# Sparse attention and two feed-forward layers on one core: paired first units, and mask, sums and scaling in other steps

## The reference

```
scores = q @ k.T / 8
mask   = scores >= the 32nd largest score of the row
attn   = softmax of the kept scores over each row
out    = attn @ v
```

```
x1 = leaky(x @ w_in1) @ w_out1     leaky(h) = max(0.01 h, h)
x2 = bump(x1 @ w_in2) @ w_out2     bump(h) = 0 below -1, h above 1, (h + 1)^2 / 4 between
```

## Time and profile before

| what | value |
|---|---|
| median of 3 runs (lowest, highest) | 1286.73 us (1286.48, 1287.85) |
| the profiled execution's own time | 1285.5 us |
| its span | 1283.6 us |
| mean granted TensorE clock | 0.949 |
| TensorE busy, share of the span | 1128.7 us, 88% |
| VectorE busy | 910.8 us, 71% |
| ScalarE busy | 700.2 us, 55% |
| GpSimd busy | 640.9 us, 50% |
| DMA | 287.12 MB, mean 224 GB/s |

### The profile page before, as it was taken

One profiled execution on the slowest core, in us unless ns is written; L12 is line 12 of the kernel. 1 busy time (PEld: TensorE's weight loads), 2 busy tenths in 40 slices (PEclk: granted clock), 3 DMA queues, 4 the chain that ended last, 5 costly groups with the idle time before them and its releaser, 6 DMA issues.

```text
span 1283.6 us, 21057 instructions
## 1 busy us (share of the span) xinstructions
PE 1128.7 (88%) x7360; PEld 1010.6 (79%) x7360; DVE 910.8 (71%) x2056; ACT 700.2 (55%) x1577; POOL 640.9 (50%) x614
## 2 busy tenths in 40 slices
PE   3334699888999989989999998999899999999998
PEld 1222488777988878878888877888788899999997
DVE  7976897989989889899996997987989201100111
ACT  4454477665657666576665754765766423322232
POOL 5454577873347454466434753543745324432343
PEclk9755699899999999999999998999999999999999
DMA  6675598777666668667866665554445667687763
GB/s 237 231 254 181 192 343 296 251 252 249 215 218 202 213 216 300 235 228 240 271 225 221 215 207 175 185 193 153 148 179 171 210 231 259 233 270 253 245 224 127
DMA packets 86504, 287.12 MB, mean 224 GB/s; under 512 B 9600, under 2 KB 13184, under 8 KB 86400
## 3 DMA queue, kind: packets, MB, share of 16 engines
q1 hardware_dynamic: 78912, 270.04, 61.5%
q10 hardware_dynamic: 7488, 15.73, 3.6%
HBM read 247.46 MB, written 38.27 MB: 223 GB/s over the span
## 4 chain that ended last, share of the span: by engine, by line
PE 62%; DVE 9%; ACT 8%; POOL 6%; issue 4%; ACTq 0%; POOLq 0%
PE ps_f L730 47%; PE ps_av L695 6%; POOL gate L575 4%; DVE top L934 3%; DVE work L937 2%; PE ps_s L651 2%; PE ps_t L672 2%; PE ps_t L651 2%; DVE part_r L961 2%; ACT probs L803 2%; ACT gate L865 1%; PE ps_t L678 1%; ACT part_o L855 1%; ACT part_r L854 1%; ACT probs L795 1%
## 5 line engine op out<-in xcount | busy, mean ns | idle before, releaser
L730 PE MATMUL ps_f<-gate,w_ring 128*128 128x384 f32 (+2 forms) x2688 | 435.2, 319 | 21.9 <-POOL gate L575 21.9
L730 PEld LDWEIGHTS ps_f<-gate,w_ring 128*128 128x128 f32 x2688 | 412.2, 192 | 40.9 <-POOL gate L575 24.6
L730 PE MATMUL ps_f<-xy,w_ring 128*128 128x384 f32 (+2 forms) x2688 | 431.0, 316 | 8.6 <-POOL xy L585 5.5
L730 PEld LDWEIGHTS ps_f<-xy,w_ring 128*128 128x128 f32 x2688 | 407.2, 190 | 26.6 <-issue 13.4
L934 DVE MAX8 top<-work 128x8 f32<-128x576 f32 x432 | 310.0, 744 | 0.1
L560 POOL TENSOR_TENSOR drop<-scores,drop 128x576 f32<-128x576 f32 x144 | 207.6, 1442 | 125.7 <-DVE drop L943 125.7
L937 DVE MATCH_REPLACE8 work<-top,work 128x576 f32<-128x576 f32 x288 | 213.6, 742 | 0.0
L575 POOL TENSOR_TENSOR gate<-part_r,gate 128x384 fp32r<-128x384 f32 (+2 forms) x112 | 101.0, 904 | 169.4 <-ACT gate L859 169.3
L965 DVE TENSOR_TENSOR y_acc<-ps_f,y_acc 128x384 f32<-128x384 f32 (+2 forms) x56 | 27.8, 497 | 208.2 <-PE ps_f L730 208.2
L961 DVE SCALAR_TENSOR_TENSOR part_r<-part_r 128x384 f32<-128x384 f32 (+2 forms) x112 | 72.3, 645 | 115.6 <-ACT part_o L855 115.3
L795 ACT ACTIVATE probs<-drop,neg_max 128x576 f32<-128x576 f32 x144 | 112.4, 781 | 62.6 <-issue 45.6
(11 more groups left out here) (79 smaller groups left out, 1290.6 us busy)
## 6 DMA issues: line engine op xcount, KB each, us to landing
w_ring<-w_split SPq DMA_DIRECT2D x412, 512.0 KB, 4.1
w_split<-w_ring SPq DMA_DIRECT2D x36, 512.0 KB, 5.5
raw<-wd SPq DMA_DIRECT2D x64, 256.0 KB, 3.9
w_split<-xy SPq DMA_DIRECT2D x28, 512.0 KB, 2.9
kq<-kqd ACTq DMA_DIRECT2D x12, 576.0 KB, 5.4
v_sb<-vd ACTq DMA_DIRECT2D x12, 320.0 KB, 3.9
kq<-kqd SPq DMA_DIRECT2D x4, 576.0 KB, 6.9
out_t<-y_acc ACTq DMA_DIRECT2D x12, 192.0 KB, 4.5
```

Source lines behind the costliest of these rows:

```text
L730: mm = pe.matmul(out, ww, xx, start=a == 0, stop=a == count - 1)
```

## The change

Six things are changed.

1. In `make_plan`, where the next unit waits for the unit just before it, it and the next one are marked `paired` and always put in one step. `feed` then runs such a pair in turn: all source blocks but the last of the first unit, all but the last of the second, then the last of the first, then the last of the second. The order of the three matmuls of a source block and their number stay.
2. GpSimd: in steps before 22 the mask goes first; the direct pieces and the low halves come one step later than before, behind mask and low_x. From step 22 on the mask keeps its place between the first and the second group.
3. SyncE: the raw loads and the stores of prepared pieces are issued one step later in its list. ScalarE's high halves stay.
4. VectorE: the items of the first four pairs close one turn earlier (before, only those of the fourth), and `close_sum` stands ahead of `find_drop`.
5. ScalarE: `normalise` goes ahead of the exponential in steps before 22; from then on it is done one step early, between the first and second group.
6. Scores of mixed items beyond tile 20 are made one step earlier.

```diff
 def score_step(it):
-    return max(0, it.first - 2) if it.first <= 20 else it.first
+    if it.first <= 20:
+        return max(0, it.first - 2)
+    return it.first - it.mixed
...
-            credit -= queue[0].ns
-            now.append(queue.pop(0))
-        cut = [a for a in range(1, len(now)) if waits_for(now[a], now[a - 1])]
-        first = cut[0] if cut else (len(now) + 2) // 3
-        second = first + (len(now) - first + 1) // 2
+            both = last is not None and waits_for(queue[0], last)
+            for u in queue[:1 + both]:
+                credit -= u.ns
+                u.paired = both
+                now.append(u)
+            last = now[-1]
+            del queue[:1 + both]
+        opens = [a for a in range(1, len(now)) if now[a].paired and waits_for(now[a], now[a - 1])]
+        first = opens[0] if opens else (len(now) + 2) // 3
+        second = first + max((len(now) - first + 1) // 2, 2 * bool(opens))
+        if second < len(now) and now[second].paired and now[second].i:
+            second += 1
...
-        if it.last + INV_LAG - (it.gp == CHUNKS[0].last_gp) == t:
+        if it.last + INV_LAG - starts_early(it.gp) == t:
...
@@ SyncE @@
-                for a in direct_pieces(s):
+                for a in direct_pieces(s - 1):
                     load_raw(a + RAW_SLOTS)
-                for i in prep_pieces(s):
+                for i in prep_pieces(s - 1):
                     store_split(i)
                     load_raw(JOB_OF[PREP[i]] + RAW_SLOTS)
...
@@ GpSimd @@
-                for u in first:
-                    event(u)
-                for a in direct_pieces(s):
-                    low_direct(a)
-                for i in prep_pieces(s)[:1]:
-                    low_piece(i)
-                if 0 <= s - MASK_LAG < TILES:
+                if s < READY[0] and s >= MASK_LAG:
                     mask(s - MASK_LAG)
                 if s - 1 in VALUES_AT and s < READY[0]:
                     low_x(VALUES_AT[s - 1])
-                for i in prep_pieces(s)[1:]:
+                for a in direct_pieces(s - 1):
+                    low_direct(a)
+                for i in prep_pieces(s - 1):
                     low_piece(i)
+                for u in first:
+                    event(u)
+                if READY[0] <= s < TILES + MASK_LAG:
+                    mask(s - MASK_LAG)
...
@@ TensorE, feed @@
+                if u.paired and u.i:
+                    return
+                open_bank(u)
+                if not u.paired:
+                    products(u, range(u.sources))
+                    return
+                other = UNITS[u.n + 1]
+                products(u, range(u.sources - 1))
+                open_bank(other)
+                products(other, range(other.sources - 1))
+                products(u, [u.sources - 1])
+                products(other, [other.sources - 1])
...
@@ ScalarE @@
+                if done and s < READY[0]:
+                    normalise(done)
                 if s < READY[0] and 0 <= s - EXP_LAG:
                     exponential(s - EXP_LAG)
...
-                if done:
-                    normalise(done)
...
+                if s + 1 in OUT_AT and s >= READY[0]:
+                    normalise(OUT_AT[s + 1])
                 for u in second:
                     event(u)
...
@@ VectorE @@
+                if shut:
+                    close_sum(shut)
+                    count += 1
                 if old:
                     dve.wait_ge(dve_step, last_top)
                     find_drop(t - 1)
                 if shut:
-                    close_sum(shut)
-                    count += 1
                     dve.wait_ge(dve_step, count)
                     invert_sum(shut)
```

More of the change, by code:

```diff
@@ L143 @@
     needs: int = -1
+    paired: bool = False
     @property
@@ L155, in ns, with sources @@
         return 3 * (CK if self.hidden else BLOCK_F) * (self.width / 2.4 + 12)
+    @property
+    def sources(self):
+        return CK if self.hidden else BLOCK_F
     @property
@@ L214, in make_plan @@
     queue, at, led = [], 0, 0
-    plan, credit = [], 0.0
+    plan, credit, last = [], 0.0, None
     for s in range(ATTENTION_STEPS + 1):
@@ L696, in values, with open_bank @@
                 mm.then_inc(av_done, 1)
-            def feed(u):
+            def open_bank(u):
                 if u.n >= BANKS:
@@ L706, in feed @@
                     pe.wait_ge(scores_copied, 2 * SCORED_EARLY)
-                count = 3 * (CK if u.hidden else BLOCK_F)
-                a = 0
                 if u.hidden and u.i == 0 and not u.layer and not u.block:
                     pe.wait_ge(x_low_done, u.chunk.last_gp + 1)
-                for g in u.pieces:
-                    if g in DIRECT:
-                        pe.wait_ge(low_split, JOB_OF[g] + 1)
-                    else:
[L715 to L731, removed]
@@ L732, in feed, with products @@
-                mm.then_inc(unit_done, 1)
+            def products(u, some):
+                for b in some:
+                    piece = 0 if u.hidden else b // F_PER_PIECE
+                    g = u.pieces[piece]
+                    if b == piece * F_PER_PIECE:
+                        if g in DIRECT:
+                            pe.wait_ge(low_split, JOB_OF[g] + 1)
+                        else:
+                            pe.wait_ge(w_loaded[g % W_SLOTS], 16 * (LOADS_BEFORE[g] + 1))
+                    m = slice((b - piece * F_PER_PIECE) * P, (b - piece * F_PER_PIECE + 1) * P)
+                    w = w_ring[:, g % W_SLOTS, :, :]
+                    if u.hidden:
+                        if u.layer and not u.block and u.i == 0:
+                            pe.wait_ge(y_low_done, Y_OF[u.chunk.n, b].y + 1)
+                        high, low, out = x_of(u.chunk, 0, b), x_of(u.chunk, 1, b), as_x(u.chunk, bank(u))
+                    else:
+                        source = GATE_OF[u.segment, b]
+                        if u.i == 0:
+                            pe.wait_ge(gate_low_done[u.layer], source.in_layer + 1)
+                        high, low, out = gate[:, 0, source.slot, 0:u.width], gate[:, 1, source.slot, 0:u.width], bank(u)
+                    end = b == u.sources - 1
+                    pe.matmul(out, w[:, 0, m], high, start=b == 0, stop=False)
+                    pe.matmul(out, w[:, 0, m], low, start=False, stop=False)
+                    mm = pe.matmul(out, w[:, 1, m], high, start=False, stop=end)
+                if end:
+                    mm.then_inc(unit_done, 1)
@@ new lines, in feed @@
+            def feed(u):
+                if u.paired and u.i:
[10 more added lines that the diff above has]
+                products(other, [other.sources - 1])
```

## The result

The changed kernel takes 1250.33 us (median of 4 runs, 1249.73 to 1252.43) beside 1287.29 us for the kernel before (4 runs, 1286.48 to 1288.33): a ratio of 0.9715, 95% interval 0.9699 to 0.9732, 37 us less. Forecast were 1249 us, 1234 to 1268. The profiled execution took 1249.73 us, with a span of 1247.7 and a mean clock of 0.953.

What follows compares the result with a forecast made beforehand. The opening was taken as latency-bound with no full engine, the rest as nearly full. Terms −30 −3.7 +4 −5 −3 = −37.7 took 1285.5 to 1247.8 us, 1249 us as a median; range 1234 to 1268.

Steps and rivals of the forecast that it cites:

- The opening: Stretch before the first main unit: start 33 us earlier, less 3 us for late raw loads, so −30 us.
- the rival of the transfers: Opening held by its transfers or raw slots, 327 of 338 GB/s: gain 17 us instead of 30, 1262 us; chance 0.15.
- the step that gave the gain to the mask's place: Opening: a weight piece ahead of the mask holds the exponential; closing item 7 earlier adds nothing at the end.
- The sum for ScalarE's chain: Opening: ScalarE's work for four tiles sums to 22.9 us, 5.7 us a turn, against 5.45 that VectorE needs.
- Lock between find_drop and low halves: Opening: VectorE and GpSimd lock each other out; costed at 0, up to 20 us; as rival 1262 us, chance 0.07.
- The 1.71 us: Opening: one find_drop beside four low halves took 1.71 us against 0.51 alone, taken as evidence of the lock.
- Pairs: Middle and end: 17 pairs hide waits ahead of last source blocks, −3.7 us, and cost +4 us on VectorE.
- catching up comes out of its own waits: VectorE, held at a pair's first addition, makes it up from existing waits; seven pairs 0 to +38 us, taken +4.
- Scaling half a step earlier: Middle: TensorE's 9.4 us of waits for scaled probabilities shrink where ScalarE was late, −5 us.
- The slower rival: Scaling between ScalarE's first and second group waits for VectorE's closing at 72 places; at 1 us each 1321 us; chance 0.04.
- Mixed scores: Middle: TensorE's 3.2 us of waits ahead of mixed scores, behind the copy of the last transposes, go: −3 us.

Runs made afterwards that it cites:

- run 3: Kernel before with both opening changes only (mask first, pieces one step later, early closings, scaling first): 1256.76 us, ratio 0.9758.
- run 2: Kernel before with early items closed one turn earlier and scaling ahead of the exponential before step 22, mask not moved: 1257.83 us, ratio 0.9773.
- run 5: Changed kernel without pairs, planner and feeding of units as before: 1244.28 us, ratio 0.9666.
- run 11: Changed kernel with pairs in the last step alone and scores of mixed items back in their old step: 1240.49 us, ratio 0.9644.
- run 12: On top of run 11, every last-step output stretch opens with a pair and the second layer puts off three source blocks: 1233.4 us, ratio 0.9588.
- run 9: Changed kernel with pairs in the last step alone and scaling from step 22 on back at the head of its own step: 1255.19 us, ratio 0.9761.
- runs 10: Changed kernel with scores of mixed items back in their old step, all else as changed: 1247.88 us, ratio 0.9695.
- run 1: Kernel before with only the mask ahead of the low halves and pieces one step later on GpSimd and SyncE before step 22: 1260.92 us, ratio 0.9797.

## Why the prediction was right

The total was right, and it came from one large term that was right in size and three small ones whose errors cancelled.

*The opening: right in size, half right in cause.* The forecast had the first unit 33 us earlier and took 3 off for raw loads: 30. It was 29.1 us earlier, at 122.57, and run 3 gives 30.8 us of time for these parts alone. The closing of item 7 came at 110.59, where 107.5 was forecast. The raw loads cost about what was foreseen: ScalarE waited for them in six pieces, 7.0 us in all and up to 2.8 at once, where 0 to 1.5 a piece was forecast. The DMA share rose to 0.78, so the rival of the transfers fell. Its ceiling had been read too low: 338 GB/s is not the busiest stretch of before, which moved 378 GB/s from 184 to 192 us. But the step that gave the gain to the mask's place, and nothing at the end to closings and scaling, failed: run 2 has 29.7 us without moving the mask. The sum for ScalarE's chain was made with both parts in, and so could not tell them apart.

*Lock between find_drop and low halves: nearly absent in the new order.* In the row of all 17 find_drops from 20 to 120 us (min, median and max in ns) the median is 508. The longest, 1274, starts at 54.80, beside low halves that a late `low_x` had pushed back to 54.48.

```profile
L979 DVE TENSOR_SCALAR drop<-scores,top x17: 504/508/1274, 22.5 to 116.1; 128x576 f32<-128x576 f32 x17
```

The term, taken at 0, holds; by the Trainium skill's rule (SBUF — State Buffer, "Who interferes with whom") that is what an order without overlap gives. The 1.71 us of the kernel before were misread in the prediction: GpSimd's four low halves end at 22.04, and what the find_drop of 22.00 ran beside is the mask of the tile before it:

```profile
22.00 1.39 POOL L560 TENSOR_TENSOR drop<-scores,drop 128x576 f32<-128x576 f32 x1
```

The find_drop of 15.79 us, 1.42 us long, is beside a low half.

*Pairs: wrong.* Forecast 3.7 won less 4 lost; measured 6.0 lost (run 5). The term that failed is the cost on VectorE, "catching up comes out of its own waits": its waits for units grew instead, by 8 to 10 us, and 7.6 to 11.1 us were lost in the attention steps. The gain there failed too: the waits for low parts of first-layer results are 6.9 us with pairs and 6.2 without. The forecast's bounds of the cost (0 to 38 us) take it in, and the value was taken too low. In the last step the waits ahead of the last block went, as forecast. That earlier blocks are late too, and keep their waits, held: they add up to 6.6 us in run 11, and run 12, with three blocks put off and more pairs, gained 7.1 us.

*Scaling half a step earlier: right in sign, some three times too small.* Forecast 5 us out of 9.4; it is worth 12.5 us (run 3 to run 5, scores included) to 15.9 us (run 9). The step that failed is reading the gain off TensorE's list of waits. That the price of a late scaling is also what the transposes hold up is a likely reading; no run separates it. Of the 15.9 us the list shows 15.0 us of waits for scaled probabilities with scaling late and none with it early, but other waits for low parts are a few us shorter then, so how the remainder divides is open. The slower rival names a wait that is real: ScalarE waits 32.9 us there in 24 pieces. It costs less than the early place gains, since the kernel is slower with the late one.

*Mixed scores: forecast 3 us, nothing.* The 3.2 us of waits went, and 11.1 us for "issue" with them, but the waits for low parts grew and the time didn't follow (runs 10, 11). The step that failed is taking a wait that goes for time that goes.

Added up in the order of the runs: 1287.5 (the kernel before beside run 3), opening −30.8, scaling and scores −12.5, pairs +6.0 gives 1250.3. Forecast were −30, −8 and +0.3. That the sum was 1 us off is chance: an error of 4.5 us one way and one of 5.7 the other.

Not tried: a fifth raw slot, to take ScalarE's waits for raw loads away.

## What to carry to other kernels

Where a chain runs round several engines and none is full, look for the ring and for every link that could stand beside another; one cut may do all of it, and two cuts do not add. Work that fills a latency pays where the engine that takes the result has nothing else to do (the end of this kernel), and costs where that engine stands in line before it with other work behind. The list of waits priced the late scaling too low and the late mixed scores too high, where the next wait took their place: try a change alone before believing its row.

## What was not expected of the hardware

A short wait can cost TensorE's granted clock as well, and the same wait does not always. In the changed kernel's last stretch the matmuls go at half rate for 3.4 us (1062.28 to 1065.73, 0.52 us each where others take 0.33), right behind a wait of 1.65 us for a gate's low part; the clock is 0.83 over 1060 to 1070 us. The 24 matmuls from 1061.63 on took 5.8 us, and 24 at full clock take 4.2. That is 1.6 us of price on top of 1.65 us of wait. The same stretch of run 5 waits 1.66 us, at 1054.64, and the clock stays at 1.00 from 1050 to 1070 us. What decides is open. The first unit shows it too: behind 1.60 us of idle its first 48 matmuls took 5.99 us in run 1 and 8.65 in run 5. Such steps are one reason why kernels with the same waits differ by 2 to 3 us. The first three rows are the changed kernel, the last run 5.

```profile
1061.63 0.44 PE L746 MATMUL ps_f<-gate,w_ring 128*128 128x384 f32 x1 [1.65 <-POOL gate L589]
...
1062.60 0.52 PE L747 MATMUL ps_f<-gate,w_ring 128*128 128x384 f32 x1
...
1060.00:1070.00 10.00, 8.37 (x39) 8.37 (x40) 0.56 (x1) 2.32 (x6) 3.88 (x5) 0.83 0.36 129
...
1054.64 5.65 PE L737 MATMUL ps_f<-gate,w_ring 128*128 128x384 f32 x31 [1.66 <-POOL gate L582]
```
